# One whole tile of score products ahead in a windowed attention kernel, with keys sent for before the inverse and a weight matrix loaded row by row

## The reference

```python
scores = scale * q @ k.T + bias          # bias = -slope[head] * distance
keep   = (key < 8) | (0 <= row - key < 96)
a      = exp(scores - max) ; a = a / (sum(a) + 1e-9)      # masked
x      = a @ v                                            # 2 x 768 x 512
gate   = sigmoid(causal depthwise conv of x, 5 taps)
x      = (gate * (x @ w_val)) @ w_out
h      = relu(x @ w_in)
gate   = sigmoid(depthwise conv of h, 3 taps)
out    = (h * gate) @ w2
```

## Time and profile before

| | us |
|---|---|
| median of three runs (lowest, highest) | 261.28 (261.14, 261.87) |
| the profiled execution's own time | 260.86 |
| its span in the trace | 259.1 |
| TensorE busy | 248.1 |
| VectorE busy | 183.4 |
| ScalarE busy | 147.8 |
| GpSimd busy | 46.8 |

### The profile page before, as it was taken

One profiled execution on the slowest core, in us unless ns is written; L12 is line 12 of the kernel. 1 busy time (PEld: TensorE's weight loads), 2 busy tenths in 40 slices (PEclk: granted clock), 3 DMA queues, 4 the chain that ended last, 5 costly groups with the idle time before them and its releaser, 6 DMA issues.

```text
span 259.1 us, 4771 instructions
## 1 busy us (share of the span) xinstructions
PE 248.1 (96%) x1702; PEld 199.7 (77%) x1702; DVE 183.4 (71%) x469; ACT 147.8 (57%) x346; POOL 46.8 (18%) x71
## 2 busy tenths in 40 slices
PE   8999989989789899999999999999999999999995
PEld 7644558888688778888888888888888888888883
DVE  0388369998989988989805969986139989990000
ACT  1061649999999854455517058855458559662100
POOL 1002255777478612000000000000000000000000
PEclk9999999999999999999999999999999999999999
DMA  6799957897976120000000000000000004004021
GB/s 204 266 341 270 287 199 202 248 239 229 271 220 202 57 74 4 0 4 0 0 0 3 0 0 0 1 3 0 0 0 3 0 0 162 3 0 162 0 115 47
DMA packets 24636, 24.69 MB, mean 95 GB/s; under 512 B 3732, under 2 KB 16532, under 8 KB 24484
## 3 DMA queue, kind: packets, MB, share of 16 engines
q1 hardware_dynamic: 23460, 23.37, 29.8%
q10 hardware_dynamic: 1152, 1.01, 1.2%
HBM read 21.03 MB, written 3.34 MB: 94 GB/s over the span
## 4 chain that ended last, share of the span: by engine, by line
PE 84%; ACT 9%; DVE 5%; issue 2%
PE ps L592 21%; PE ps L594 21%; PE ps L593 21%; PE ps L478 9%; ACT prob L732 6%; PE ps L559 3%; DVE prob L982 3%; PE ps L525 2%; PE ps L563 2%; ACT probT L739 2%; PE ps L493 2%; PE ps L489 1%; DVE probT L989 1%; DVE xT L1005 1%; ACT Wh L720 0%
## 5 line engine op out<-in xcount | busy, mean ns | idle before, releaser
L732 ACT ACTIVATE prob<-prob,low 128x232 f32<-128x232 f32 (+1 forms) x96 | 44.2, 465 | 4.9 <-DVE low L982 4.8
L1010 DVE SCALAR_TENSOR_TENSOR g<-xT,cw,g 128x512 f32<-128x512 f32 x48 | 34.7, 787 | 1.6 <-ACT g L767 1.6
L838 ACT ACTIVATE h<-ps 128x512 f32<-128x512 f32 x24 | 14.0, 596 | 31.2 <-PE ps L594 31.1
L982 DVE CUSTOM_DVE_ANT_0 prob<-ps,bias 128x232 f32<-128x232 f32 x80 | 28.0, 388 | 1.5 <-PE ps L525 1.5
L559 PE MATMUL ps<-probT,v_new 128*64 128x128 f32 x192 | 19.3, 280 | 6.5 <-ACT probT L739 6.5
L592 PE MATMUL ps<-gh,Wh 128*128 128x512 f32 x64 | 24.9, 389 | 0.0
L593 PE MATMUL ps<-gl,Wh 128*128 128x512 f32 x64 | 24.9, 389 | 0.0
L594 PE MATMUL ps<-gh,Wl 128*128 128x512 f32 x64 | 24.9, 389 | 0.0
L592 PE MATMUL ps<-hghA,w2h 128*128 128x512 f32 x64 | 24.9, 389 | 0.0
L593 PE MATMUL ps<-hglA,w2h 128*128 128x512 f32 x64 | 24.9, 389 | 0.0
L594 PE MATMUL ps<-hghA,w2l 128*128 128x512 f32 x64 | 24.9, 389 | 0.0
(11 more groups left out here) (110 smaller groups left out, 590.1 us busy)
## 6 DMA issues: line engine op xcount, KB each, us to landing
q_rows<-in_q SPq DMA_DIRECT2D x12, 256.0 KB, 4.3
kW<-in_k SPq DMA_DIRECT2D x12, 256.0 KB, 5.4
v_new<-in_v SPq DMA_DIRECT2D x12, 240.0 KB
invT<-inv_turned SPq DMA_DIRECT2D x20, 128.0 KB, 3.4
out<-xT SPq DMA_DIRECT2D x5, 512.0 KB, 2.8
w<-in_w SPq DMA_DIRECT2D x8, 256.0 KB, 9.3
v_old<-in_v SPq DMA_DIRECT2D x10, 192.0 KB
prob<-in_wval SPq DMA_DIRECT2D x1, 1024.0 KB, 4.9
```

What stands on the lines that cost most here:

```text
L732: act.activation(part, part, ACT.Exp, scale=-1.0, bias=low[:, t % 2, i:i + 1], accum_out=total[:, t % 2, i, 0:1]).then_inc(exp_done, 1)
L838: act.activation(h_cols(m, c), pieces(HB(m), c), ACT.Relu).then_inc(relu_done, 1)
L982: dve.tensor_tensor_reduce(prob[:, t % 2, i, cols], SC(f, e)[:, i % HH // 2, cols], table, -SCALE, 3.0e38, ALU.add, ALU.min, low[:, t % 2, ...
L1010: dve.scalar_tensor_tensor(out=pieces(g[:, m, :], c), in0=x_cols(m, c, tap - PAD1), scalar=cw1[:, m, tap:tap + 1], in1=pieces(g[:, m, :], ...
```

## The change

- TensorE: `qk` is cut into `qk_half`, and the loop is now `turn(t, 0)`, `turn(t, 1)`, `qk(t+2)`, `pv(t)`.
- VectorE: all of `score(1)` is done ahead of the loop. A tile is then: copy 1, inverse, copy 3, turn of the inverse, the early step if there is one, eight `score(t+2)`, `take_x(t)`.
- ScalarE: three exponentials of the next tile's scores are done ahead; a tile is two copies, five exponentials of t+1 and three of t+2.
- VectorE's early convolution steps move from the tiles 8, 9, 10 to 6, 8, 10.
- SyncE: queries and keys of tile t+4 are issued ahead of `send_inverse(t)`, no longer behind it and the values. Only three rows of `w2` are loaded ahead of the loop, and one at the end of each tile 0 to 4.
- GpSimd: `split_w2` takes rows 0 and 1 in tile 0, one row each in tiles 1 to 4, and rows 6 and 7 in tile 5.

```diff
-EARLY_STEPS = {t: 1 for t in range(TAPS_FROM + 3, TILES - 1)}
+EARLY_STEPS = {t: 1 for t in (X_SPLIT_FROM, X_SPLIT_FROM + 2, TILES - 2)}
+W2_FIRST = 3
+EXP_AHEAD = 3
+W2_ROWS = {0: (0, 1), 1: (2,), 2: (3,), 3: (4,), 4: (5,), 5: (6, 7)}
...
-                for k in range(FT):
+                for k in range(W2_FIRST):
                     load_w2(k)
                 for t in range(TILES):
+                    if t + RING < TILES:
+                        load_q(t + RING)
+                        load_k(t + RING)
                     send_inverse(t)
                     if t >= 1 and t - 1 + RING < TILES:
                         load_v(t - 1 + RING)
-                    if t + RING < TILES:
-                        load_q(t + RING)
-                        load_k(t + RING)
                     spread_inverse(t)
+                    if t + W2_FIRST < FT:
+                        load_w2(t + W2_FIRST)
...
-                    if t < FT // 2:
-                        split_w2(2 * t)
-                        split_w2(2 * t + 1)
+                    for k in W2_ROWS.get(t, ()):
+                        split_w2(k)
...
                 for t in range(TILES - 1):
-                    if t >= 1:
-                        qk(t + 1)
                     for f in range(HALVES):
                         turn(t, f)
+                    if t + 2 < TILES:
+                        qk(t + 2)
                     pv(t)
...
+                for i in range(EXP_AHEAD):
+                    exp_of(1, i)
                 for t in range(TILES - 1):
-                    exp_of(t + 1, 0)
-                    exp_of(t + 1, 1)
                     copy_t0(t, 0)
                     copy_t0(t, 2)
-                    exp_of(t + 1, 2)
-                    exp_of(t + 1, 3)
-                    for i in range(HH, H):
+                    for i in range(EXP_AHEAD, H):
                         exp_of(t + 1, i)
+                    if t + 2 < TILES:
+                        for i in range(EXP_AHEAD):
+                            exp_of(t + 2, i)
...
+                for i in range(H):
+                    score(1, i)
                 for t in range(TILES - 1):
-                    if t >= 1:
-                        take_x(t - 1)
-                    score(t + 1, 0)
-                    score(t + 1, 1)
+                    copy_t1(t, 1)
                     inverse(t)
-                    score(t + 1, 2)
+                    copy_t1(t, 3)
                     turn_inverse(t)
-                    copy_t1(t, 1)
-                    score(t + 1, 3)
-                    copy_t1(t, 3)
-                    for i in range(HH, H):
-                        score(t + 1, i)
                     for _ in range(EARLY_STEPS.get(t, 0)):
                         early_conv1(next_step)
                         next_step += 1
-                take_x(TILES - 2)
+                    if t + 2 < TILES:
+                        for i in range(H):
+                            score(t + 2, i)
+                    take_x(t)
```

More of the change, by code:

```diff
@@ L511, in _, with qk_half @@
             product_W(CT + 1)
+            def qk_half(t, f):
+                slot = t % RING
+                if f == 0:
+                    pe.wait_ge(q_in[slot], landed(t))
+                    pe.wait_ge(k_in[slot], landed(t))
+                    pe.wait_ge(k_window, k_windows(t))
+                if t >= 1:
+                    pe.wait_ge(score_done, H * (t - 1) + HH * (f + 1))
+                for i in range(HH):
+                    pair, rows = 2 * f + i // 2, slice(i % 2 * D, i % 2 * D + D)
+                    keys = kW[rows, slot, pair, OLD if first_of_batch(t) else 0:KEYS]
+                    last = pe.matmul(SC(f, i % 2)[:, i // 2, OLD if first_of_batch(t) else 0:KEYS], q_rows[rows, slot, pair, :], keys,
+                                     start=True, stop=True)
+                last.then_inc(qk_done, 1)
             def qk(t):
[L515 to L518, removed]
                 for f in range(HALVES):
-                    if t >= 1:
[L521 to L527, removed]
+                    qk_half(t, f)
             def turn_bank(t, j):
```

## The result

The changed kernel takes 269.53 us in the median (267.64 to 272.24, four executions), against 261.21 for the kernel before on the same chip: a ratio of 1.0289, interval 1.0233 to 1.0346. The medians are of all executions, while a ratio compares those in the fast state alone (272.24 was in the slow one), so it differs from the quotient of the medians. The forecast was 264.5, with a range up to 268.2. The direction and the kind of cause were right; the size was not, and the time lies above the range.

What follows compares the result with a forecast made beforehand. The prediction took the order between four nearly full engines, one ring through both copies and hand-overs, as the bound. 260.86 + 0.6 (loop) + 2.6 (late keys) = 264.1, plus 0.4 for the median: 264.5 us, range 259.0 to 268.2.

Steps and rivals of the forecast that it cites:

- A tile in the new order: Tile loop: the old ring is cut, a new one through `take_x` gives 4.92 us a tile against 5.03.
- The ring over `take_x`: Eight scores, `take_x`, hand-over to TensorE, transposes, first half of the score products, back to VectorE's scores: 4.92 us.
- Faster: Rival: the ring over `take_x` isn't the bound, 4.7 us a tile, early steps hide for 0.5 more: 259.4 us; chance 0.27.
- The first tile: Loop entrance: `turn(1, 1)` at 42.8 against 41.1 before; the new order pays 1.7 us once to get ahead.
- The loop's end with nothing else late: From the loop to the next stage's first product: 89.7 against 89.14 before, so +0.6 us.
- plus 1.1: Loop: early convolution steps in tiles 6 and 8 stand ahead of the scores and add 1.1 us.
- The convolution step meets GpSimd: Rival: VectorE's step slows beside GpSimd's multiply, twice 1.0 in the ring: 266.5 us with late keys; chance 0.08.
- SyncE and the keys: SyncE's serial loop needs 6.2 us in tiles 1 to 4, 5.7 in 5 and 6; tile 11's keys late by 2.6.
- The fixed part: SyncE's tile without L: keys, two spreads, a row of `w2` and queries, 2.6 us with that row.
- L: SyncE: time from the inverse's write until its landing, taken as 3.59 us; break-even 3.15, range top at 4.2.
- GpSimd's way: `split_w2(7)` waits for its row, `scale_x(4)` and tile 9's window queue behind it: about the same lateness, not on top.
- The rule against the change: Inverse not reported before keys issued ahead have landed: L near 5.0, last keys 11 us late; left out of the sum.

Runs made afterwards that it cites:

- the first experiment: Changed kernel's new order on TensorE, ScalarE and VectorE, with SyncE and GpSimd as in the kernel before, all `w2` rows loaded ahead of the loop: 263.98 us, ratio 1.0118.
- keys between: The first experiment's kernel with queries and keys issued directly behind `send_inverse`, ahead of the values: 263.91 us, ratio 1.0102.
- the kernel with all that helped: New compute order, `w2` ahead of the loop, keys between inverse and values (tile 0: ahead of inverse), early steps in tile 10: 261.69 us, ratio 1.0029.
- with fills: The first experiment's kernel with zero products in TensorE's waits for `take_x` (tiles 1, 7, 9) and keys (tiles 7, 8): 263.60 us, ratio 1.0083.

## Why the prediction was right or wrong

**A tile in the new order: right.** The ring over `take_x` was summed to 4.92, and the score products start 4.92 apart. The rival "Faster", which decides from a period under 4.85, falls with it.

**The first tile: right.** `turn(1, 1)` came at 43.02 for a forecast 42.8, behind a pause of 1.53.

**The loop's end with nothing else late: near.** The term "plus 1.1" for two early steps measured 1.3 in the trace of the first experiment and 1.2 in the changed kernel's (0.73 and 0.5); the runs say 1.7 to 2.0 for taking them out, with executions that scatter by more than that. The rival "The convolution step meets GpSimd" was right that the step of tile 6 meets GpSimd, and its price of twice 1.0 was not: the step begins before its scores are there, and the one of tile 8 took 0.71. The rest of the term holds: with windows in time and the steps moved out the loop ends 0.4 before the old one, and the two steps make that some 0.8 behind it, where 0.6 was forecast.

**SyncE and the keys: the mechanism right, the size wrong; this is the step that failed.** "Late by 2.6 us" was 6.2 in the profiled execution: `qk(9)` starts at 71.94 with the windows in time, would start at 72.8 here (entrance 0.1 later, step of tile 6 0.7), and started at 79.05. Three parts of the step are off:
- The fixed part, taken as 2.6, was 3.0 in the mean of the four tiles up to the keys of tile 9 (27.68 from 44.33 to 72.01, less 15.64 of L). The `w2` issue takes 0.61 and not the 0.45 that was estimated from an issue "of the same kind", the queries mostly 0.43 to 0.61 and not 0.39, some 0.04 lies between any two, and once SyncE stood 0.44 in front of the queries (57.61 to 58.05). Issues that stall, as the keys at 72.01 for 1.46, have no term at all, though the earlier trace rows shows keys that took 1.03; this one came behind row 7 and only made the later tiles later.
- L, taken as 3.59, was 3.63 in the mean of the first six tiles (2.86 to 4.35 over seven), but 3.91 in the four that decide. With the fixed part this made the tiles 7.26, 6.88, 6.37 and 7.17 long where 6.2 was written: the keys of tile 9 left 2.8 late against the forecast's own 69.2, and row 7 of `w2` 2.4 late against its 68.4.
- The lateness was read at tile 11, by its keys, and GpSimd's way was put down as "about the same lateness, not on top". It is the one that decided, in tile 9. With the forecast's own 68.4 for row 7, the 4.2 that it took to land and the 3.9 of GpSimd behind it, that window is finished at 76.5. `qk(9)` is wanted at 72.4 (82.8 less two periods and the 0.6 of the step in tile 8): 4.1 late, not 2.6.

**GpSimd as the second way: right in kind.** It ends in `qk(9)` beside SyncE's, as the run with row 7 a tile later shows, and it was the longer one by some 0.9 us.

**What no term held: TensorE's clock behind a wait.** In the earlier trace rows it is 1.00, so a wait was priced at its own length. In the changed kernel the waits of 1.52 and 2.56 us are each followed by a stretch at 1.2 GHz, from 65.2 to 68.7 and from 78.9 to 82.3, while an idle time of 1.69 at 75.8 is not. `qk(7)` to `qk(8)` took 70.63 - 64.21 = 6.42 against 4.71 with the windows in time (keys between), `qk(9)` to `qk(10)` 85.55 - 79.05 = 6.50 against 4.92. Only the second is paid for. SyncE's issues from 58.05 to those of tile 9 at 72.01 follow one another with nothing but landings between them, and by the code they need of TensorE only what was done by 60. So without the first wait and the first fall `qk(9)` would only have waited longer for the same window.

With this the 8.8 of the profiled execution are made up: the ring 0.43 less, the entrance 0.14, the two steps 0.73 and 0.51, the late window of tile 9 6.24, the clock behind it 1.58; together 8.77. Against the forecast's start of the last stage, 92.3, the measured 97.92 is 5.6 later: 2.5 for SyncE's longer loop up to row 7, 1.6 for the clock, and 1.5 because tile 9 decided and not tile 11.

That a wait for keys is the cause of a fall is argued from the order of the rows, and it is not a rule: behind 1.96 in the run with keys between the clock held. For the pause in tile 1 it is shown, by the table above.

**The rule against the change: not seen.** With 512 KB of queries and keys issued directly ahead of the write, its reporting took 3.63 in the mean, no longer than with keys behind it (3.17 to 4.87 in the run with only that moved) or before (2.75 to 4.81). The prediction took the rule to mean that the inverse is reported only when the keys ahead of it have landed. Here it was reported first: the keys issued at 58.47 had landed at 63.3, the write issued behind them, at 58.93, was reported by 62.41, when the spread follows.

```profile
63.30 0.51 POOL L413 COPY kW<-kW 128x384 f32<-128x384 f32 x1 [1.99 <-DMA kW<-in_k]
```

The Trainium skill ("DMA: Bandwidth & Descriptors", queues, rings and completion order) speaks of the earlier writes of the same DMA engine. No row here tells which of the 16 engines a transfer used, so this refutes the estimate of 5.0, not the page.

**The range** was taken from the uncertainty of L alone. Its top, 268.2 at L = 4.2, left out that a wait can be followed by 1.6 us of lost clock, that the fixed part of SyncE's sum, written without a doubt, had two terms too short and none for stalls, and that the other way could be the longer one.

## What to carry to other kernels

Before a transfer is moved into an engine's serial loop, add up every issue of that loop with the duration of the very same line, and put the moved one where the engine only waits: the place of five issues of 0.61 us was worth 2 to 4 us here. Follow each way to the tile in which it bites, since two ways that seem equal can bite in different tiles. In a loop in which TensorE is just full, a wait for data can cost 1.6 us more than its length, since products behind it may run at half clock; a wait that hides behind a longer one costs nothing. And when a ring is only 0.1 us a tile shorter than the old one, what stands in it once (an entrance, a convolution step beside GpSimd) decides; taking such steps out of the old ring gained 1.1 us, while the new order, at its best, gained none that can be told.

## What the runs showed of the hardware

- **Short pauses and the clock.** The pause of 1.53 us in tile 1 is in every kernel of the new order that doesn't fill or stretch it. With rows ahead and keys behind, the clock held in the profiled execution; with rows ahead and keys in front it fell:

```profile
42.18 0.23 PE L552 MATMUL ps<-ident,prob 64*104 64x64 f32 x1 [1.53 <-issue]
...
42.67 3.15 PE L529 MATMUL ps<-kW,q_rows 64*128 64x232 f32 x16
```

  The next score products came 6.53 later and not 4.92, so one fall costs 1.6 us. The same pause falls on either side from execution to execution (four of ten in the kernel with all that helped), filled it hardly ever does (one of twelve), and at 1.87 nearly always (nine of ten). What decides in one execution stays open. The scatter of the new order (2.2 to 5.6 us in its kernels with all rows ahead; 1.8 to 2.8 in the kernel before, one execution of 359.52 aside) is only in part the clock: with fills, nine executions without a fall still spread over 2.6 us.
- **A step beside GpSimd.** VectorE's 128x512 step took 1.32 us beside GpSimd's split, 1.71 (first experiment) and 1.73 beside its multiply, and 0.71 to 0.75 alone.
- **Issues differ by kind.** On SyncE: 0.32 for a small value issue, 0.43 keys, 0.56 the inverse's write, 0.61 a row of `w2` behind the spreads and 0.35 to 0.47 inside the wait, 1.26 the pair of spreads; and now and then one issue takes 1.0 to 1.6.
